# Where VectorE adds the last two output units to Y at the end of an odd step: behind both turned tiles' remainders, or each ahead of one

## The chip, the cores and the metric

One core of a Trainium2 chip runs the whole program: TensorE (PE) multiplies, VectorE (DVE), ScalarE (ACT) and GpSimd (POOL) work on its operands and results, SyncE (SP) issues the loads and stores. The metric is the device time of one execution in microseconds; three runs stand for a kernel by their median.

## The reference, cut to what matters

Attention over 4 batches of 8 heads, each 576 tokens by 64, with a second answer from a memory matrix, mixed by a gate; then two MLPs over the 2304 tokens.

```python
scores = scale * q @ k.T;  scores = where(causal, -1e9, scores)
a = exp(scores - scores.max(-1)); a /= a.sum(-1) + 1e-9
local = a @ v
q_p = where(q > 0, q, exp(q) - 1) + 1
mem_out = (q_p @ M_prev) / (q_p @ z_prev + 1e-6)
x = g * mem_out + (1 - g) * local            # g = sigmoid(beta), by head
x = (sigmoid(x @ w_gate) * (x @ w_val)) @ w_out      # 2304 x 512 -> 1536 -> 512
h = x @ w_in;  out = (h * clip(h + 3, 0, 6) / 6) @ w_out2   # 512 -> 2048 -> 512
```

## The kernel before, in words

**Numbers in two parts.** Operands of most products are cut in a part of reduced width, `hi`, and the remainder, `lo`; a product is then three matmuls (hi hi, hi lo, lo hi). ScalarE writes hi, and VectorE or GpSimd writes lo, which needs hi first.

**Pairs and steps.** The heads go in 16 pairs. A pair is two steps, p = 0 (the even step) and p = 1 (the odd one), and each step has five slots, i = 0 to 4. Pairs 0 to 4 run without MLP work (`lead`). From pair 5 on, each step carries, beside the attention of its pair, half of a quarter of the first MLP for an older batch: the function `step` on each engine. `walk` calls it: pairs 5 to 7 in a loop, pair 8 by itself with `cut` set, pairs 9 to 11 in the loop, pair 12 with `cut`, 13 and 14 in a loop, 15, and then a step pair without scores. The rest of the first MLP follows alone, and the second MLP after it.

**Turned tiles.** A head's probabilities lie by query rows. PE transposes tile i of them into PSUM (`turn_head`), ScalarE copies it to `pt_hi` (`move_hi`), and VectorE writes `pt_lo` = PSUM - `pt_hi` (`move_lo`, line 1157, counted by the semaphore `lo_done`). The table `MOVE[p][i]` says which tiles go in which slot. In the odd step's last slot, i = 4, these are tiles 2 and 3 of the even head (128x384 and 128x512); below they are m2 and m3. Tile 4 (128x320, "old") follows in slot 0 of the next step; below m4. All five must be there before PE multiplies by V (`times_v`).

**Units of the first MLP.** `FILL[p][i]` gives PE's MLP work of a slot: gate units G0 to G5, value units V0 to V5, output units O0 to O7; "T" is the turning of tile 3. A unit covers 288 tokens and accumulates in one PSUM bank. O0 to O7 take banks 6 and 7 in turn (`out_bank`), and so do the units before and after them. VectorE adds each output unit from PSUM to the running sum `Y` (line 1348, semaphore `f_y`); below s6 and s7 are those of O6 and O7. Slot (1, 4) on PE is O6, turn of tile 3, O7, scores of the next head's tile 0, turn of tile 4. The next step begins with scores of tile 1, and then G0 and G1, `times_mem`, `times_v`.

**What G0 and G1 wait for** (lines 705 to 709): G0 (t = 0) needs s6, because it takes the bank of O6, and also m2; G1 (t = 1) needs s7 and m3:

```python
if t < 2: pe.wait_ge(f_y, OU * (r + 1) - 1 + t)
if t < 2 and n is not None: pe.wait_ge(lo_done, piece_head(n - 1, 0, t + 2) + 1)
```

**Order on the engines.** It is the order of the code; each engine works its own stream in order. ScalarE in slot (1, 4): a wait for the staged weights at the end of the slot before (`high_w`, line 941), hi of tile 2, exp of tile 4 of the odd head, hi of tile 3. VectorE in slot (1, 4): mask and maximum of tile 4 of the odd head (line 1209), m2, m3, in pairs 8 and 12 also two parts of `x_lo` (`cut_x`, line 1224, each behind ScalarE's x_hi), s6, s7. The next step begins on VectorE with the mask of tile 0, the row scales (lines 1163 to 1169) and m4.

The weights arrive in a ring of three tiles: SP loads, ScalarE takes hi, GpSimd takes lo (`low_w`, line 509), which frees the tile. SP's queue in the odd step holds the loads of the next q and k, which wait for `q_s` (line 1125), ahead of the load of w_val that ScalarE waits for.

Of the kernel before, what the change touches and what calls it, by code (L numbers as in the profile page):

```python
# [31 lines left out]
def attention_and_mlps(nc, qk_t, q_n, v_n, mem, z, beta, w_gate, w_val, w_out1, w_in, w_out2, out):  # L32
# [14 lines left out]
    OU = 2 * DT  # L47
# [101 lines left out]
    with ExitStack() as ctx:  # L149
# [15 lines left out]
        def out_bank(j, alone):  # L165
            return j if alone else MLP + j % 2
# [79 lines left out]
        def softmax_tiles(p, i):  # L246
            return {2: (2, 3), 3: ()}.get(i, (i,)) if p == 0 else (i,)
# [66 lines left out]
        def tokens(c):  # L314
            return slice(c * HALF, (c + 1) * HALF)
# [804 lines left out]
        def _(dve):  # L1120
            def low_q(n, p):
                qk = qk_home(2 * n + p)
                dve.wait_ge(q_hi_done, 2 * n + p + 1)
                low = slice(D, P)
                dve.scalar_tensor_tensor(q_s[p][low, 0:S], qk[low, 0, :], SCALE, q_s[p][low, 0:S].bitcast(F32),  # L1125
                                         ALU.mult, ALU.subtract).then_inc(q_ready, 1)
# [15 lines left out]
            def move_lo(n, p, kind, i, r):  # L1142
                nn = n if p else n - 1
                if kind == "phi":
                    dve.wait_ge(hi_done, piece_phi(n, i) + 1)
                    cols = slice(0, (QT - 1) * P) if i == 0 else slice((QT - 1) * P, S)
                    src = ps[:, TURN, 0:(QT - 1) * P] if i == 0 else ps[:, turn_bank(r, 0), P:P + TAIL]
                    dst, hi = phit_lo[:, cols], phit_hi[:, cols]
                else:
                    odd = 1 - p if kind == "head" else p  # L1150
                    nn = nn if kind == "head" else n - 1
                    dve.wait_ge(hi_done, whole_bank(nn, odd, i))
                    rows = qrows[i]
                    src = ps[:, turn_bank(r, i), 0:(i + 1) * rows].rearrange("p (k c) -> p k c", c=rows)
                    cols = slice(i * P, i * P + rows)
                    hi, dst = [t[:, 0:i + 1, cols] for t in pt_main]
                dve.tensor_tensor(dst, src, hi.bitcast(F32), ALU.subtract).then_inc(lo_done, 1)  # L1157

            def row_scales(n, p):
                u, o, nn = 2 * n + p, 1 - p, (n if p else n - 1)  # L1160
                q5 = slice(0, QT)
                dve.wait_ge(exped, QT * u)
                dve.tensor_scalar(rsum_e[o][:, q5], rsum[o][:, q5], 1e-9, None, ALU.add).then_inc(sum_e, 1)
                dve.wait_ge(sum_e, u)
                dve.reciprocal(rinv[o][:, q5], rsum_e[o][:, q5]).then_inc(sum_r, 1)
                dve.wait_ge(sum_r, u)
                if known(nn, 1):
                    dve.wait_ge(normed, QT * (u - 2))
                dve.tensor_scalar(rscale[o][:, q5], rinv[o][:, q5], gate_1mg[:, bass.ds(u - 1, 1)], None, ALU.mult).then_inc(rinved, 1)  # L1169

            def phi_sum(n):
                dve.wait_ge(q_exped, n + 1)
                dve.wait_ge(relued, n + 1)
                flat = [t[:, :, :].rearrange("p t c -> p (t c)") for t in (phi, q_exp)]
                dve.scalar_tensor_tensor(flat[0], flat[1], 1.0, flat[0], ALU.min, ALU.add).then_inc(phied, 1)
# [18 lines left out]
            def low_m(n):  # L1194
                dve.wait_ge(m_hi_done, 2 * (n + 1))
                for j in two:
                    dve.tensor_tensor(m_hl[j][own(j), other(j)], m_st[own(j), :], m_hl[j][own(j), own(j)].bitcast(F32), ALU.subtract).then_inc(m_ready, 1)

            def mask_tile(n, p, j):
                u = 2 * n + p  # L1200
                if known(n, 1):
                    dve.wait_ge(turned, whole_bank(n - 1, p, j))
                dve.wait_ge(scored, QT * u + j + 1)
                settled(dve, settled_dve)
                dst = prob[p][:, p_off[j]:p_off[j] + width[j]]
                bias = mask[:, (QT - 1 - j) * P:(QT - 1 - j) * P + width[j]]
                if j == QT - 1:
                    dst, bias = [t.rearrange("p (a c) -> p a c", a=2) for t in (dst, bias)]
                dve.tensor_tensor_reduce(dst, score(p, j), bias, -1.0, MOST, ALU.add, ALU.min, nmax[p][:, j:j + 1]).then_inc(maxed, 1)  # L1209

            def x_sum(n, p, q):
                dve.wait_ge(xl_done, 2 * n + p - 1)
                dve.tensor_tensor(x_new[own(p), bass.ds(q, 1), :].rearrange("p a c -> p (a c)"), head_out(0, S)[own(p), :],
                                  x_low[own(p), :], ALU.add).then_inc(x_done, 1)
# [76 lines left out]
            def step(n, p, old, turn, scoring, r, b, q, cut):  # L1291
                alone = not (scoring or old)

                def moves(i, part=slice(None)):
                    for kind, j in MOVE[p][i][part]:
                        if (old if kind == "old" else turn):
                            move_lo(n, p, kind, j, r)

                for i in range(QT):
                    for j in softmax_tiles(p, i) if scoring else ():  # L1300
                        if j < QT - 1 or p == 1:
                            mask_tile(n, p, j)
                    if i == 0 and turn:
                        row_scales(n, p)
                    if (p, i) not in ((0, 3), (0, 4)):
                        moves(i)
                    elif i == 4:
                        moves(i, slice(0, 1))
                    if i == 1 and old:
                        x_sum(n, p, q)  # L1310
                    if p == 0 and scoring and i == 1:
                        low_q(n, 1)
                        phi_sum(n)
                    if p == 1 and turn and i == 3:
                        low_m(n)
                    if cut is not None and p == 1 and i in CUT_X:
                        cut_x(cut, CUT_X[i])
                    if p == 0 and scoring and i == QT - 2:
                        phi_scales(n)
                    for unit in FILL[p][i]:  # L1320
                        if unit[0] == "V":
                            g = int(unit[1])
                            here = slice(None), g // 2, tokens(g % 2)
                            if alone:
                                dve.wait_ge(f_gout, GV * r + g + 2)
                            else:
                                dve.wait_ge(f_sig, FQ * r + g // 2 + 1)
                            dve.wait_ge(f_val, GV * r + g + 2)
                            dve.tensor_tensor(h_val[here], h_gate[here], ps[:, unit_bank(GV + g, alone), 0:HALF], ALU.mult).then_inc(f_vout, 1)
                            if g == 0:  # L1330
                                moves(i)
                            else:
                                hidden_lo(r, g - 1)
                            if g == 2:
                                moves(i, slice(1, None))
                            if g == GV - 1:
                                if scoring:
                                    phi_scaled(n)
                                hidden_lo(r, g)
                        if unit[0] == "O":  # L1340
                            j = int(unit[1])
                            if j == 0:
                                dve.wait_ge(y_zero, B)
                            y = Y[:, j // 2, bass.ds(b * S + (j % 2) * HALF, HALF)]
                            dve.wait_ge(f_out, OU * r + j + 2)
                            if known(r, 1):
                                dve.wait_ge(f_y, OU * r + j + 1)
                            dve.tensor_tensor(y, ps[:, out_bank(j, alone), 0:HALF], y, ALU.add).then_inc(f_y, 1)  # L1348
                    if p == 0 and scoring and i == QT - 2:
                        mask_tile(n, p, QT - 1)  # L1350
                    if p == 1 and scoring and i == 1 and not is_last(n, p):
                        low_q(n + 1, 0)

            walk(dve, lead, step)


# [42 lines left out]
```

## Time and profile before

| what | value |
|---|---|
| median of 3 runs | 1146.13 us (1146.13 to 1151.61) |
| profiled execution | 1150.61 us |
| its span, first to last instruction | 1148.8 us |
| PE busy | 1099.7 us, 96% |
| VectorE busy | 580.5 us, 51% |
| ScalarE busy | 560.8 us, 49% |
| GpSimd busy | 496.9 us, 43% |
| DMA, mean | 71 GB/s |

The pairs with MLP work beside them take up the time from about 100 to 600 us of the span, some 43 us each; the second MLP starts at about 740 us. The profiled execution is 4.48 us longer than the median of the three. Busy time is that of instructions; idle time of an engine is shown with what ended it.

### The profile page before, as it was taken

To read this page: it belongs to the slowest core of one execution; us is meant where nothing else is said; L and a number is where in the kernel's file an instruction comes from. 1 tells how busy PE (TensorE), PEld (TensorE's weight loads), DVE (VectorE), ACT (ScalarE), POOL (GpSimd) and SP (SyncE) were. 2 spreads that over 40 slices of the span, in tenths; PEclk is the share of its full clock that TensorE was granted. 3 is DMA by queue.
4 is the path that set the end of the run, shared out by engine and by line. 5 is a ranking of instruction groups with operands and counts; after the bars stand their busy time and mean duration, and the time that the engine had idled before them with its cause. 6 is when DMAs were issued, how large, how long until landed. Compare 5 with 4: busy or idle time off the path is not lost.

```text
span 1148.8 us, 21924 instructions
## 1 busy us (share of the span) xinstructions
PE 1099.7 (96%) x6928; PEld 1020.3 (89%) x6928; DVE 580.5 (51%) x1313; ACT 560.8 (49%) x1259; POOL 496.9 (43%) x517
## 2 busy tenths in 40 slices
PE   4998999998999998999999999999999999999998
PEld 3677999998999998999999999899999999999996
DVE  5987656756756757756734333532323232232321
ACT  5777666675766676666753333222323232232322
POOL 5889557655756655656643444993000000000000
PEclk8999999999999999999999999899999999999999
DMA  7542432442343343343222233440000000000000
GB/s 177 138 116 51 124 99 72 115 107 61 92 114 89 99 109 87 90 117 90 57 65 74 83 82 83 125 124 28 27 0 27 0 27 0 0 27 0 27 0 27
DMA packets 100195, 81.36 MB, mean 71 GB/s; under 512 B 7729, under 2 KB 85553, under 8 KB 100145
## 3 DMA queue, kind: packets, MB, share of 16 engines
q1 hardware_dynamic: 100144, 80.77, 26.4%
q8 instruction: 22, 0.36, 0.1%
q14 instruction: 29, 0.23, 0.1%
HBM read 76.03 MB, written 4.72 MB: 70 GB/s over the span
## 4 chain that ended last, share of the span: by engine, by line
PE 81%; DVE 5%; issue 4%; DMA 3%; ACT 3%; POOL 1%; SPq 1%; DVEq 0%; ACTq 0%; POOLq 0%
PE ps L595 77%; DMA stage<-w_val 3%; PE ps L636 3%; PE ps L650 1%; DVE q_s L1125 1%; ACT pt_hi L913 1%; DVE Y L1348 1%; ACT prob L956 1%; SPq L355 1%; DVE prob L1209 1%; POOL prob L522 1%; DVE phi L1191 0%; DMA stage<-w_gate 0%; DVE znorm_e L1181 0%; DVE znorm L1179 0%
## 5 line engine op out<-in xcount | busy, mean ns | idle before, releaser
L595 PE MATMUL ps<-x_hi,WG 128*128 128x288 f32 x1536 | 326.2, 299 | 12.8 <-DVE Y L1348 11.7
L595 PEld LDWEIGHTS ps<-x_hi,WG 128*128 128x128 f32 x1536 | 252.4, 188 | 17.0 <-DVE pt_lo L1157 9.9
L595 PE MATMUL ps<-x_lo,WG 128*128 128x288 f32 x768 | 226.8, 295 | 0.0
L595 PE MATMUL ps<-c_hi,W 128*128 128x384 f32 x768 | 213.4, 340 | 2.9 <-DVE c_lo L1360 2.9
L509 POOL TENSOR_TENSOR WG<-stage,WG 128x512 fp32r<-128x512 f32 x96 | 129.1, 1363 | 125.1 <-ACT WG L941 125.1
L595 PE MATMUL ps<-W,g_hi 128*128 128x512 f32 x576 | 179.0, 391 | 0.0
L595 PE MATMUL ps<-h_hi,WO 128*128 128x288 f32 x768 | 166.2, 299 | 5.6 <-DVE Y L1348 5.6
L1365 DVE SCALAR_TENSOR_TENSOR g_raw<-g_raw,ps 128x384 f32<-128x384 f32 x96 | 53.2, 554 | 222.0 <-ACT g_raw L1101 222.0
L1101 ACT ACTIVATE g_raw<-ps 128x384 f32<-128x384 f32 x96 | 47.3, 492 | 212.3 <-PE ps L595 212.3
L595 PEld LDWEIGHTS ps<-c_hi,W 128*128 128x128 f32 x768 | 142.0, 190 | 8.0 <-DVE c_lo L1360 4.3
L522 POOL TENSOR_SCALAR prob<-prob,rscale 128x128 f32<-128x128 f32 (+4 forms) x160 | 109.1, 701 | 91.2 <-DVE rscale L1169 91.2
L595 PEld LDWEIGHTS ps<-x_lo,WG 128*128 128x128 f32 x768 | 145.0, 189 | 0.4
L595 PEld LDWEIGHTS ps<-h_hi,WO 128*128 128x128 f32 x768 | 127.4, 189 | 7.0 <-DVE Y L1348 6.6
L595 PE MATMUL ps<-c_lo,W 128*128 128x384 f32 x384 | 130.1, 339 | 0.0
L595 PEld LDWEIGHTS ps<-W,g_hi 128*128 128x128 f32 x576 | 106.9, 188 | 18.3
L956 ACT ACTIVATE prob<-prob,nmax 128x128 f32<-128x128 f32 (+4 forms) x160 | 95.9, 601 | 51.8 <-DVE nmax L1209 51.2
L595 PE MATMUL ps<-W,g_lo 128*128 128x512 f32 x288 | 113.7, 395 | 0.0
L595 PE MATMUL ps<-h_lo,WO 128*128 128x288 f32 x384 | 113.7, 296 | 0.0
L1209 DVE CUSTOM_DVE_ANT_0 prob<-ps,mask 128x128 f32<-128x128 f32 (+4 forms) x160 | 85.8, 538 | 11.3 <-PE ps L595 6.6
L1157 DVE TENSOR_TENSOR pt_lo<-ps,pt_hi 128x128 fp32r<-128x128 f32 (+4 forms) x120 | 58.6, 489 | 60.3 <-ACT pt_hi L913 60.2
L1367 DVE SCALAR_TENSOR_TENSOR g_lo<-g_raw,g_hi 128x384 fp32r<-128x384 f32 x96 | 55.9, 582 | 57.6 <-ACT g_hi L1105 57.6
L595 PE MATMUL ps<-k_hi,q_s 128*128 128x128 f32 (+2 forms) x192 | 73.7, 391 | 9.7 <-DVE k_lo L1131 8.2
(104 smaller groups left out, 1829.6 us busy)
## 6 DMA issues: line engine op xcount, KB each, us to landing
stage<-w_out SPq DMA_DIRECT2D x64, 256.0 KB, 2.8
qk_st<-qk_t SPq DMA_DIRECT2D x54, 288.0 KB, 4.3
stage<-w_gate SPq DMA_DIRECT2D x48, 256.0 KB, 3.2
stage<-w_val SPq DMA_DIRECT2D x48, 256.0 KB, 3.0
out<-y_out SPq DMA_DIRECT2D x6, 768.0 KB, 3.5
qn_st<-q_n SPq DMA_DIRECT2D x16, 256.0 KB, 3.1
stage<-w_in SPq DMA_DIRECT2D x16, 256.0 KB, 2.7
v_st<-v_n SPq DMA_DIRECT2D x12, 256.0 KB, 2.7
```

Source lines behind the costliest of these rows:

```text
L355: sp.dma_start(home[half * D:half * D + D, :, :], qk_t[bass.ds(u, 1), :, :, :].rearrange("a d c s -> (a d) c s")).then_inc(ld_qk if home i ...
L509: pool.tensor_tensor(lo, stage[k % NST][:, :], hi.bitcast(F32), ALU.subtract).then_inc(w_done, 1)
L522: pool.tensor_scalar(t, t, rscale[o][:, i:i + 1], 1.0, ALU.mult, ALU.mult).then_inc(normed, 1)
L595: return pe.matmul(o, l, r, start=start, stop=stop, skip_group_check=True)
L636: last = pe.transpose(ps[:, turn_bank(r, i), k * rows:(k + 1) * rows], prob[odd][0:rows, p_off[i] + k * P:p_off[i] + (k + 1) * P], ident[0 ...
L650: last = pe.transpose(ps[:, TURN if j == 0 else turn_bank(r, 0), o:o + rows], phi[0:rows, t, :], ident[0:rows, 0:rows])
L956: act.activation(dst, dst, ACT.Exp, scale=-1.0, bias=nmax[p][:, j:j + 1], accum_out=rsum[p][:, j:j + 1]).then_inc(exped, 1)
L1101: act.activation(g_raw[f % 2][:, :], ps[:, f % 4, 0:CH], ACT.Relu, bias=3.0).then_inc(b_relu, 1)
L1157: dve.tensor_tensor(dst, src, hi.bitcast(F32), ALU.subtract).then_inc(lo_done, 1)
L1209: dve.tensor_tensor_reduce(dst, score(p, j), bias, -1.0, MOST, ALU.add, ALU.min, nmax[p][:, j:j + 1]).then_inc(maxed, 1)
L1365: dve.scalar_tensor_tensor(raw, raw, 6.0, ps[:, f % 4, 0:CH], ALU.min, ALU.mult).then_inc(b_g, 1)
L1367: dve.scalar_tensor_tensor(g_lo[f % 4][:, :], raw, 1.0 / 6.0, g_hi[f % 4][:, :].bitcast(F32), ALU.mult, ALU.subtract).then_inc(b_lo, 1)
```

## The change

In slot i = 4 of the odd step VectorE no longer writes m2 and m3 ahead of the two sums. It adds s6, writes m2, adds s7, writes m3. The move stands behind the sum in the loop over `FILL`, and so also behind `cut_x` in pairs 8 and 12, where it stood ahead of it. Where no head is turned in that slot (the step pair behind the last pair, and the rest) nothing differs.

```diff
-                    if (p, i) not in ((0, 3), (0, 4)):
+                    if (p, i) not in ((0, 3), (0, 4), (1, 4)):
                         moves(i)
-                    elif i == 4:
+                    elif (p, i) == (0, 4):
                         moves(i, slice(0, 1))
...
                             dve.tensor_tensor(y, ps[:, out_bank(j, alone), 0:HALF], y, ALU.add).then_inc(f_y, 1)
+                            if j >= OU - 2:
+                                moves(i, slice(j - (OU - 2), j - (OU - 2) + 1))
```

VectorE, the end of an odd step in the inner loop, from the mask of tile 4 to the loop's branch, before:

```order
 L1209 ISA prob_88,nmax_93<-ps,mask 128x576
 L1209 ISA nmax_93 128x1
-L1152 REGISTER_ALU
-L1157 TENSOR_TENSOR pt_lo<-ps,pt_hi 128x3x128
-L1152 REGISTER_ALU
-L1157 TENSOR_TENSOR pt_lo<-ps,pt_hi 128x4x128
-L1345 REGISTER_ALU
-L1348 ISA
-L1348 TENSOR_TENSOR Y<-ps,Y 128x288
```

The two remainders (m2 is 128x3x128, m3 is 128x4x128) stand ahead of the first sum; the second follows it. Now:

```order
+L1345 REGISTER_ALU
+L1348 ISA
+L1348 TENSOR_TENSOR Y<-ps,Y 128x288
+L1152 REGISTER_ALU
+L1157 TENSOR_TENSOR pt_lo<-ps,pt_hi 128x3x128
+L1345 REGISTER_ALU
+L1348 ISA
+L1348 TENSOR_TENSOR Y<-ps,Y 128x288
+L1152 REGISTER_ALU
+L1157 TENSOR_TENSOR pt_lo<-ps,pt_hi 128x4x128
```

The sum of O6 has moved up past both remainders, and the sum of O7 past m3; m3 is the last instruction of the step.

VectorE, the same slot in pairs 8 and 12, where x is cut (one piece of the difference; line 1224 is the second x_lo):

```order
-L1152 REGISTER_ALU
-L1157 TENSOR_TENSOR pt_lo<-ps,pt_hi 128x3x128
-L1152 REGISTER_ALU
-L1157 TENSOR_TENSOR pt_lo<-ps,pt_hi 128x4x128
 L1223 REGISTER_ALU
 L1224 TENSOR_TENSOR x_lo<-x_new,x_hi 128x576
```

Both remainders leave their place ahead of the two x_lo and go, in turn with the sums, behind them. Nothing moves on PE, ScalarE, GpSimd or SP.

## Rows read from the trace of the kernel before

**Rows 1.** The page, costliest group: count | busy, mean ns | idle before, releaser.
```profile
L595 PE MATMUL ps<-x_hi,WG 128*128 128x288 f32 x1536 | 326.2, 299 | 12.8 <-DVE Y L1348 11.7
```

**Rows 2.** PE's timeline at the end of pair 6: start, duration, [idle before <- releaser].
```profile
185.82 0.29 PE L595 MATMUL ps<-h_hi,WO 128*128 128x288 f32 x1
...
187.46 0.30 PE L595 MATMUL ps<-h_hi,WO 128*128 128x288 f32 x1
...
188.53 0.28 PE L595 MATMUL ps<-k_lo,q_s 128*128 128x256 f32 x1
189.65 0.40 PE L595 MATMUL ps<-x_hi,WG 128*128 128x288 f32 x1 [0.84 <-DVE Y L1348]
...
192.80 0.29 PE L595 MATMUL ps<-x_hi,WG 128*128 128x288 f32 x1
```

**Rows 3.** VectorE's timeline at the same place.
```profile
185.12 0.75 DVE L1209 CUSTOM_DVE_ANT_0 prob<-ps,mask 128x576 f32<-128x576 f32 x1
...
187.21 0.56 DVE L1157 TENSOR_TENSOR pt_lo<-ps,pt_hi 128x384 fp32r<-128x384 f32 x1 [1.33 <-ACT pt_hi L913]
188.45 0.69 DVE L1157 TENSOR_TENSOR pt_lo<-ps,pt_hi 128x512 fp32r<-128x512 f32 x1 [0.68 <-ACT pt_hi L913]
189.06 0.81 DVE L1348 TENSOR_TENSOR Y<-ps,Y 128x288 f32 x2
189.97 0.29 DVE L1209 CUSTOM_DVE_ANT_0 prob<-ps,mask 128x128 f32<-128x128 f32 x1
```

**Rows 4.** ScalarE's timeline at the same place.
```profile
186.17 0.63 ACT L941 ACTIVATE WG<-stage 128x512 fp32r<-128x512 f32 x1 [2.12 <-DMA stage<-w_val]
186.70 0.47 ACT L913 ACTIVATE pt_hi<-ps 128x384 fp32r<-128x384 f32 x1
```

**Rows 5.** PE's timeline: the first product of G0 behind other pairs.
```profile
145.27 0.60 PE L595 MATMUL ps<-x_hi,WG 128*128 128x288 f32 x1 [2.39 <-DVE Y L1348]
...
279.44 0.39 PE L595 MATMUL ps<-x_hi,WG 128*128 128x288 f32 x1 [0.96 <-DVE Y L1348]
...
454.33 0.40 PE L595 MATMUL ps<-x_hi,WG 128*128 128x288 f32 x1 [1.03 <-DVE Y L1348]
...
498.24 0.39 PE L595 MATMUL ps<-x_hi,WG 128*128 128x288 f32 x1 [1.85 <-DVE Y L1348]
```

**Rows 6.** VectorE's timeline: m2 and m3 of pair 5, m2 of pair 13.
```profile
142.83 0.56 DVE L1157 TENSOR_TENSOR pt_lo<-ps,pt_hi 128x384 fp32r<-128x384 f32 x1 [2.88 <-ACT pt_hi L913]
144.07 0.69 DVE L1157 TENSOR_TENSOR pt_lo<-ps,pt_hi 128x512 fp32r<-128x512 f32 x1 [0.68 <-ACT pt_hi L913]
...
495.80 0.56 DVE L1157 TENSOR_TENSOR pt_lo<-ps,pt_hi 128x384 fp32r<-128x384 f32 x1 [2.44 <-ACT pt_hi L913]
```

**Rows 7.** VectorE's timeline, the end of pair 8 (x is cut here) and the next step's start.
```profile
278.84 0.82 DVE L1348 TENSOR_TENSOR Y<-ps,Y 128x288 f32 x2
282.26 0.29 DVE L1209 CUSTOM_DVE_ANT_0 prob<-ps,mask 128x128 f32<-128x128 f32 x1 [2.60 <-issue]
```

**Rows 8.** PE's timeline behind pair 8: products by V, and a later gate unit.
```profile
283.80 0.58 PE L595 MATMUL ps<-pt_hi,v_hl 128*128 128x128 f32 x2 [0.29 <-DVE pt_lo L1157]
...
304.12 0.40 PE L595 MATMUL ps<-x_hi,WG 128*128 128x288 f32 x1 [0.48 <-DVE h_val L1329]
```

**Rows 9.** VectorE's timeline, the end of pair 12 (x is cut here) and the next step's start.
```profile
453.74 0.81 DVE L1348 TENSOR_TENSOR Y<-ps,Y 128x288 f32 x2
454.47 0.28 DVE L1209 CUSTOM_DVE_ANT_0 prob<-ps,mask 128x128 f32<-128x128 f32 x1
```

**Rows 10.** Stretches: length, busy of PE, PEld, DVE, ACT, POOL, granted clock, DMA share.
```profile
145.00:148.00 3.00, 2.73 (x11) 2.74 (x12) 2.03 (x10) 1.75 (x4) 1.08 (x3) 0.53 0.36 100
...
499.00:503.00 4.00, 4.00 (x31) 3.93 (x30) 0.96 (x4) 3.03 (x8) 3.31 (x6) 1.00 0.05 14
```

**Rows 11.** The chain that ended last, merged: PE's first pieces behind pairs 5 and 13.
```profile
145.27 10.86 PE ps L595 x66
...
498.24 9.37 PE ps L595 x66
```

## The prediction

> **What bounds the kernel now.** I read the page first: PE is busy for 96% of the span (the table above), so only a change that removes PE's idle time or its work can shorten anything. The page's costliest group, the products of x with the gate and value weights, sat idle for 12.8 us before its instructions, and 11.7 of that was ended by a sum to Y [rows 1]. I then went through PE's timeline of the eleven pairs, 5 to 15. Each has exactly one such wait, at the first product of G0: 0.84 us behind pair 6 [rows 2], 2.39, 0.96, 1.03 and 1.85 behind pairs 5, 8, 12 and 13 [rows 5], the other six between 0.34 (pair 15) and 1.05. In a plain pair it is the only wait PE has in 43 us, so the pair is as long as PE's work and this wait.
>
> **What the wait is, in pair 6.** PE ends the scores of tile 1 at 188.81 (188.53 + 0.28) and starts G0 at 189.65 [rows 2]. VectorE is free at 185.87, when the mask of tile 4 is done (185.12 + 0.75), and then stands idle for 1.33 us until ScalarE's hi of tile 2 is there; it writes m2 from 187.21 to 187.77, waits 0.68 us for hi of tile 3, writes m3 from 188.45 to 189.14, and only then does s6 [rows 3]. ScalarE is late because it waited 2.12 us for the staged w_val; its hi of tile 2 ends at 187.17 [rows 4]. But O6 was done long before: its last matmul ends at 186.11, and that of O7 at 187.76 [rows 2]. Both sums wait in line behind remainders that wait for ScalarE. A sum takes 0.41 us from start to start (0.81 for two, 0.46 for the last), and PE starts 0.13 us after s6's end.
>
> **Part 1: s6 and m2 ahead of G0, plain pairs.** After the change s6 runs from about 186.15 to 186.6, in the idle 1.33 us, at no cost. m2 keeps its start, 187.21, since it waits for ScalarE, and ends at 187.77; with 0.13 us for the signal G0 may start at 187.90. PE comes at 188.81. The wait of 0.84 us goes whole, with 0.9 us to spare. The same holds where m2 starts about 2.4 us ahead of G0. Two pairs are different. Behind pair 5 PE comes at 142.88 (145.27 - 2.39) and m2 ends at 143.39 [rows 5, 6]: G0 at 143.52, 0.64 us of wait remain, 1.75 are gained. Behind pair 13 PE comes at 496.39 and m2 ends at 496.36: 0.10 remain, 1.75 are gained. In pair 15 the wait of 0.34 goes.
>
> Sum: 11.7 for all eleven, less 0.96 and 1.03 for pairs 8 and 12, less the 0.64 and 0.10 that remain: **9.0 us** gained in nine pairs.
>
> **Part 2: G1.** It now waits for m3. s7 can start when O7 is done, at 187.80, and ends by 188.26; m3 starts as before at 188.45, with ScalarE's hi, and ends at 189.14. G1 starts when G0's work is done: the two units fill 189.65 to 193.09, less a little at the end [rows 2], so a unit is 1.6 us, and G1 starts at 188.81 + 1.6 = 190.4. That is 1.3 us after m3. In pair 5 m3 ends at 144.76 and G1 comes at 143.52 + 1.6 = 145.1: closer, still nothing. Cost zero; the cover is G0's own work.
>
> **Part 3: what stands behind m3.** The mask of tile 0 started at 189.97, behind s7; now it follows m3, at about 189.2, 0.77 us sooner [rows 3]. PE is 0.84 us sooner. So VectorE, and ScalarE's exp and GpSimd's scaling that hang on it, keep step with PE to within 0.1 us. Only behind pairs 5 and 13 does PE run ahead of them by a further 1.0 us. What such a lag costs can be read behind pair 8, where the mask comes 2.8 us after G0's start (282.26 against 279.44), not 0.3 as in pair 6: PE loses 0.29 and 0.48 us there [rows 7, 8]. A lag of 1.0 against one of 2.5 that costs 0.77: between 0 and 0.3 us each. I take 0: pair 6, with the mask 0.3 us behind G0, loses nothing, and the lag here is nearer to it than to pair 8's.
>
> **Part 4: pairs 8 and 12, a loss.** Here m2 and m3 were written while ScalarE made x_hi, in time that VectorE otherwise waits. They now come behind both x_lo. In pair 8, s6 still starts at 278.84 [rows 7]. m2 is queued between it and s7 (0.48 us from start to start) and m3 behind s7 (0.61): VectorE ends the step 1.1 us later. Behind that the next mask comes 1.1 us later, and m4 too, so the products by V start at 284.9 in place of 283.80 [rows 8]. They waited already, so PE loses the full **1.1 us**; G0's own 0.5 us is inside that. The work through GpSimd and the staging that ends in the wait at 304.12 is later by the same 1.1 and adds nothing. In pair 12 the mask starts 0.14 us behind G0 and not 2.8 (454.47 against 454.33) [rows 5, 9], so 1.1 us more leaves it well short of pair 8's lag, and only G0's part counts: s6 starts at 453.74, m2 ends 0.94 us later at 454.68, G0 at 454.81 in place of 454.33: **0.5 us**. Ends of this term: 0.5 each (1.0) to 1.1 each (2.2); I take 1.6.
>
> **Part 5: TensorE's clock.** Behind the longest wait, 2.39 us at pair 5, the granted clock is 0.53 from 145 to 148, that is near the lower level of 1.2 GHz; behind 1.85 us at pair 13 it stays at 1.00, 2.4 GHz [rows 10]. The same 66 matmuls take 10.86 us behind pair 5 and 9.37 behind pair 13 [rows 11]. So a wait cut to 0.64 us may also give back 1.5 us. I leave it out of the forecast: the profiled execution is 4.5 us longer than the median, and such a slow stretch is one of the few things in it that could be absent from the two equal runs at 1146.13.
> The Trainium skill, page "TensorE: Matmul & The Clock Gate", Part 1: The HAM clock gate, says that the default state is throttled and that activity releases it. The trace agrees here (0.53, then 0.92 and 1.00), and by that rule the 1.5 us would be gained.
>
> **Sum.** 9.0 - 1.6 = **7.4 us**. Against the profiled execution that is 1150.6 - 7.4 = 1143.2 (1141.7 with the clock). Against the median, 1146.13 - 7.4 = **1138.7 us**, 0.65% less.
>
> **Rivals.**
> *The long waits are not in the median run.* The waits behind pairs 5 and 13 exceed the usual 0.85 us by 1.5 and 1.0. In the shorter runs ScalarE's weights may come on time there. Then these two give 0.85 each and not 1.75: 7.4 - 1.8 = 5.6, **1140.5 us**. For it: the 4.5 us between the executions. Against it: pair 5 is the first with MLP work, so its wait may be in every run.
> *The clock as well*: 8.9, **1137.2 us**.
> *The wait moves on.* PE runs ahead and meets ScalarE or GpSimd one unit later, at the copy of G0 or the products by V. If half of every wait came back, 4.5 - 1.6 = 2.9: **1143.2 us**. Against it: 1.3 us of slack at G1.
> *Slower: m3 is held by O7.* VectorE now stands at s7 until O7 is done, with m3, the next mask, the row scales and all of GpSimd's scaling in line. The Trainium skill, same page, Architectural detail, says that VectorE's queue is strict FIFO; the rows below agree in that no sum overtook a remainder. It decides where O7 ends more than about 0.3 us after ScalarE's hi of tile 3: then m3 ends later than s7 did. If that held in all eleven pairs with pair 8's price of 1.1 us, 12 us would be lost: **1158 us**. Against it: O7 ends at 187.76 and m3's operand is there at 188.4; only in pair 15 are the two about even.
> *No effect*: G0 is in truth held by something that s6 only happens to end with. 1146.1. Against it: PE follows s6 by 0.13 us.
>
> **How the numbers follow.** Forecast 0.56; without the long waits 0.17; with the clock 0.10; the wait moves on 0.10; slower 0.04; no effect 0.03. A measurement of this kernel tells some 0.5% (5.7 us, 1140.4) from no change. The forecast, the clock and about a third of the rival at 1140.5 lie below that: faster 0.72; same 0.24; slower 0.04. The range: down to the clock's case with the loss of Part 4 at its low end and a little over (1137.2 - 0.6, and 1 us for the spread of runs), 1135.6; up to the wait that moves on, 1143.2, so 1143.6.
>
> **What the profile after would show.** On PE's timeline G0 follows the scores without a wait behind nine pairs (0.6 behind pair 5 at most), and pairs are 0.8 us shorter. On VectorE one sum stands in the former idle time ahead of m2, and m3 keeps its distance to ScalarE's hi. Behind pair 8 the wait before the products by V is about 0.9 us, and behind pair 12 G0 waits 1.5. I am wrong if a new wait shows at G1, at `times_v` in plain pairs, or if the sum of O6 ends behind hi of tile 2.

## The result, and the profile after

The changed kernel takes 1140.53 us (median of 10 runs, 1137.47 to 1143.73), the kernel before, beside it, 1147.58 us (median of 10, 1145.89 to 1151.61). The ratio is 0.9931, 95% interval 0.9917 to 0.9944. By the medians that is 7.05 us less, by the ratio 7.9, where 7.4 was forecast; the time itself is 1.8 us above the forecast 1138.7, mostly because the kernel before is now 1.45 us above the 1146.13 that the forecast started from. In two later comparisons the kernel before took 1146.83 and 1147.75 us.

The page after, the busy time of the engines and PE's costliest group, to be read against [rows 1]:

```profile
span 1139.1 us, 21924 instructions
...
PE 1099.2 (96%) x6928; PEld 1020.8 (90%) x6928; DVE 587.2 (52%) x1313; ACT 560.2 (49%) x1259; POOL 498.6 (44%) x517
...
L595 PE MATMUL ps<-x_hi,WG 128*128 128x288 f32 x1536 | 325.5, 298 | 3.9 <-DVE pt_lo L1157 2.7
```

Of 12.8 us of idle time before these products 3.9 are left, and what ends them is no longer a sum to Y but a remainder: 2.7 us, which are two waits, 1.28 and 1.39 us, behind pairs 8 and 12.

At the end of pair 6, VectorE after (start, duration, idle before), to be read against [rows 3]:

```profile
182.87 0.46 DVE L1348 TENSOR_TENSOR Y<-ps,Y 128x288 f32 x1 [0.39 <-PE ps L595]
183.70 0.56 DVE L1157 TENSOR_TENSOR pt_lo<-ps,pt_hi 128x384 fp32r<-128x384 f32 x1 [0.37 <-ACT pt_hi L913]
184.50 0.46 DVE L1348 TENSOR_TENSOR Y<-ps,Y 128x288 f32 x1 [0.25 <-PE ps L595]
184.94 0.69 DVE L1157 TENSOR_TENSOR pt_lo<-ps,pt_hi 128x512 fp32r<-128x512 f32 x1
185.88 0.29 DVE L1209 CUSTOM_DVE_ANT_0 prob<-ps,mask 128x128 f32<-128x128 f32 x1 [0.25 <-issue]
```

s6 stands alone in the former idle time, m2 waits for ScalarE as before, s7 waits 0.25 us for O7, and m3 follows it. m3 starts 1.24 us behind m2, as before (188.45 against 187.21 [rows 3]), so s7 does not delay it. PE at the same place, and then at V4, the first unit of the odd step, and at the G0 behind pair 7:

```profile
185.14 0.27 PE L595 MATMUL ps<-k_lo,q_s 128*128 128x256 f32 x1
185.25 0.30 PE L595 MATMUL ps<-x_hi,WG 128*128 128x288 f32 x1
...
207.05 0.30 PE L595 MATMUL ps<-x_hi,WG 128*128 128x288 f32 x1
...
227.01 0.30 PE L595 MATMUL ps<-x_hi,WG 128*128 128x288 f32 x1
```

G0 starts 0.11 us after the start of the last score matmul; it had been 1.12 us, 188.53 to 189.65 [rows 2]. The same two units, V4 and the G0 behind pair 7, before:

```profile
211.55 0.30 PE L595 MATMUL ps<-x_hi,WG 128*128 128x288 f32 x1
...
232.74 0.39 PE L595 MATMUL ps<-x_hi,WG 128*128 128x288 f32 x1 [1.05 <-DVE Y L1348]
```

From the G0 behind pair 6 to the one behind pair 7 it was 232.74 - 189.65 = 43.09 us and is now 227.01 - 185.25 = 41.76.

Where the time went, from the start of V4 in the odd step of one pair to the start of V4 in the next pair (each row holds the odd step, the wait at the G0 behind it, and the next even step):

| behind pair | before, us | after, us | difference | wait in the row before |
|---|---|---|---|---|
| 5 | 46.62 | 42.76 | -3.86 | 2.39, and a slower clock behind it |
| 6 | 42.89 | 41.77 | -1.12 | 0.84 |
| 7 | 43.09 | 41.76 | -1.33 | 1.05 |
| 8 (x cut) | 47.25 | 47.96 | +0.71 | 0.96 |
| 9 | 43.42 | 42.48 | -0.94 | 0.74 |
| 10 | 42.79 | 41.76 | -1.03 | 0.74 |
| 11 | 42.92 | 41.78 | -1.14 | 0.89 |
| 12 (x cut) | 45.22 | 47.08 | +1.86 | 1.03 |
| 13 | 43.90 | 41.78 | -2.12 | 1.85 |
| 14 | 42.87 | 41.77 | -1.10 | 0.86 |
| 15 | 39.65 | 39.27 | -0.38 | 0.34 |

The sum is -10.45. The stretch ahead of it was 0.48 us longer in this execution and the one behind it 0.3, which leaves the 9.7 us between the spans of 1148.8 and 1139.1.

Of the wait of 2.39 us behind pair 5, 0.10 is left in this execution (the last score matmul ends at 143.28, G0 starts at 143.38), too short for a bracket. Both columns hold slow stretches of TensorE's clock, 1.5 us each: before in rows 5 and 8, after in rows 8 and 12. That of row 8 stands behind another wait, at O4 in slot 2, which the change doesn't touch; more on it below.

The pairs where x is cut lost. VectorE behind pair 8 before, m3 and the two x_lo that follow it at once:

```profile
276.90 0.69 DVE L1157 TENSOR_TENSOR pt_lo<-ps,pt_hi 128x512 fp32r<-128x512 f32 x1 [1.53 <-ACT pt_hi L913]
277.51 1.42 DVE L1224 TENSOR_TENSOR x_lo<-x_new,x_hi 128x576 fp32r<-128x576 f32 x2
```

And after, to be read against [rows 7] as well:

```profile
271.63 1.43 DVE L1224 TENSOR_TENSOR x_lo<-x_new,x_hi 128x576 fp32r<-128x576 f32 x2 [2.66 <-ACT x_hi L948]
272.97 0.45 DVE L1348 TENSOR_TENSOR Y<-ps,Y 128x288 f32 x1
273.34 0.55 DVE L1157 TENSOR_TENSOR pt_lo<-ps,pt_hi 128x384 fp32r<-128x384 f32 x1
273.80 0.45 DVE L1348 TENSOR_TENSOR Y<-ps,Y 128x288 f32 x1
274.17 0.68 DVE L1157 TENSOR_TENSOR pt_lo<-ps,pt_hi 128x512 fp32r<-128x512 f32 x1
277.12 0.29 DVE L1209 CUSTOM_DVE_ANT_0 prob<-ps,mask 128x128 f32<-128x128 f32 x1 [2.27 <-issue]
```

VectorE idles for 2.66 us until x_hi is there, time in which both remainders used to be written, and writes them behind it. PE, after, behind pairs 8 and 12 (G0, the products by V, G0), with [rows 5, 8]:

```profile
273.94 0.40 PE L595 MATMUL ps<-x_hi,WG 128*128 128x288 f32 x1 [1.28 <-DVE pt_lo L1157]
...
278.66 0.58 PE L595 MATMUL ps<-pt_hi,v_hl 128*128 128x128 f32 x2 [0.64 <-DVE pt_lo L1157]
...
446.43 0.45 PE L595 MATMUL ps<-x_hi,WG 128*128 128x288 f32 x1 [1.39 <-DVE pt_lo L1157]
```

The waits grew from 0.96, 0.29 and 1.03 us. Behind pair 12 the clock fell as well in this execution. The stretches after (length, busy of PE, PEld, DVE, ACT, POOL, granted clock, DMA share, GB/s):

```profile
446.00:450.00 4.00, 3.57 (x15) 3.58 (x16) 2.77 (x11) 2.12 (x5) 1.46 (x4) 0.58 0.00 0
450.00:454.00 4.00, 4.00 (x28) 3.91 (x28) 0.00 (x0) 2.27 (x7) 3.83 (x6) 0.99 0.00 0
```

0.58 is near 0.5, the lower level of 1.2 GHz. The step behind that G0 takes 23.44 us, and 21.91 before: 1.53 of the 1.86.

### The profile page after: what moved, and what is told of

Read it like the earlier page. It is cut to its first block, busy times and chain, and to the rows that moved or that the text cites. A ratio compares the mean times of both kernels' runs of the same rounds, so it can differ in the third digit from the quotient of the medians.

```text
span 1139.1 us, 21924 instructions
## 1 busy us (share of the span) xinstructions
PE 1099.2 (96%) x6928; PEld 1020.8 (90%) x6928; DVE 587.2 (52%) x1313; ACT 560.2 (49%) x1259; POOL 498.6 (44%) x517
## 4 chain that ended last, share of the span: by engine, by line
PE 85%; DVE 4%; issue 3%; ACT 2%; POOL 2%; DMA 1%; DVEq 0%; SPq 0%; ACTq 0%; POOLq 0%
PE ps L595 81%; PE ps L636 3%; PE ps L650 1%; POOL prob L522 1%; DMA stage<-w_gate 1%; DVE prob L1209 1%; DVE phi L1191 0%; DMA stage<-w_val 0%; POOL WO L509 0%; ACT pt_hi L913 0%; DVE znorm_e L1181 0%; DVE Y L1348 0%; DVE znorm L1179 0%; ACT prob L956 0%; DVE q_s L1125 0%
## 5 line engine op out<-in xcount | busy, mean ns | idle before, releaser
L1369 DVE SCALAR_TENSOR_TENSOR g_lo<-g_raw,g_hi 128x384 fp32r<-128x384 f32 x96 | 60.4, 630 | 57.5 <-ACT g_hi L1105 57.5
L1329 DVE TENSOR_TENSOR h_val<-h_gate,ps 128x288 f32<-128x288 f32 x96 | 42.9, 447 | 74.7 <-PE ps L595 53.9
```

Of the source, the lines that this page charges most:

```text
L1369: dve.scalar_tensor_tensor(g_lo[f % 4][:, :], raw, 1.0 / 6.0, g_hi[f % 4][:, :].bitcast(F32), ALU.mult, ALU.subtract).then_inc(b_lo, 1)
```

## The experiments

**Theory A**: the gain is PE's wait at G0 in nine plain pairs, each worth its idle time plus a fixed part; the change loses in pairs 8 and 12. **Rivals**: the cut pairs cost nothing (B); the gain is steadier loads and a steadier clock in one execution or the other, not the order (C).

### Only the plain pairs, only the cut pairs

```diff
-                    if (p, i) not in ((0, 3), (0, 4), (1, 4)):
+                    if (p, i) not in ((0, 3), (0, 4), (1, 4)) or ((p, i) == (1, 4) and cut is not None):
...
-                            if j >= OU - 2:
+                            if j >= OU - 2 and cut is None:
```

> The order of the change in the plain pairs only; pairs 8 and 12, where x is cut, keep the order of before (m2, m3, x_lo, x_lo, s6, s7). Theory A: the gain is PE's wait at G0 in nine plain pairs, each the idle time of its row plus some 0.26 us (a stream of matmuls overlaps by 0.16 us and starts again 0.10 us late), and the two cut pairs lose 0.7 and 0.3 us, and 1.5 more where the clock falls. Then this kernel is 1 to 2.5 us shorter than the change and 8 to 9.5 us shorter than before, and behind pairs 8 and 12 G0 waits 0.96 and 1.03 us again as before. Rival B: the cut pairs cost nothing and the change's gain is all in place already: same as the change within 0.3 us.

Measured: 1137.32 us (4 runs) beside 1146.83 before (19 runs), ratio 0.9917 (0.9889 to 0.9946): 9.5 us less, at the upper end of the 8 to 9.5 expected. Its interval overlaps that of the change, so by itself it doesn't show that the cut pairs cost anything. The second kernel has `cut is None` and `cut is not None` exchanged:

> The complement: the order of the change only in pairs 8 and 12, the plain pairs as before. Theory A: 1.0 us longer than before, up to 2.5 where the clock falls behind one of them; every plain pair keeps its wait (0.74 to 1.05 us) and its odd half of 21.0 us. Rival C (the gain comes from steadier loads or a steadier clock over the whole stretch and not from the order in each pair): shorter than before by some us, with plain pairs changed too.

Measured: 1150.23 us (10 runs), ratio 1.0030 (1.0014 to 1.0047): 3.4 us more, clear of no change, and more than the 1.0 to 2.5 expected. The two add to -6.1, the whole change is -7.05. The rows of pairs 6 and 7 (V4 to V4) are 41.78 us each in the first kernel and 42.87 and 43.07 in the second, as after and before. So B and C both fall: the order in the plain pairs is the gain, and the cut pairs cost, which the second kernel shows. G0 behind pairs 8 and 12 in the first, and behind pair 12 in the second with the clock of the stretch behind it:

```profile
272.79 0.39 PE L595 MATMUL ps<-x_hi,WG 128*128 128x288 f32 x1 [1.03 <-DVE Y L1348]
...
445.84 0.39 PE L595 MATMUL ps<-x_hi,WG 128*128 128x288 f32 x1 [0.94 <-DVE Y L1348]
```

```profile
453.70 0.40 PE L595 MATMUL ps<-x_hi,WG 128*128 128x288 f32 x1 [1.39 <-DVE pt_lo L1157]
```

```profile
455.00:460.00 5.00, 5.00 (x29) 4.93 (x29) 1.08 (x5) 3.29 (x8) 4.09 (x7) 0.74 0.00 0
```

In the second kernel's trace the cut pairs are 0.68 us (pair 8) and 1.84 us (pair 12, 1.52 of it clock) longer than before, 2.5 in all; the other 0.9 us of its median isn't placed. A lower clock over the runs may be part of it: the mean granted clock of its ten runs is 0.9920, that of the nineteen before 0.9939, an estimated 2.2 us of the span where the cut pairs of the trace have 1.52, but single runs scatter from 0.987 to 0.997.

### Both sums first

```diff
-                            if j >= OU - 2:
-                                moves(i, slice(j - (OU - 2), j - (OU - 2) + 1))
+                            if j == OU - 1:
+                                moves(i)
```

> Both sums first and then both remainders (s6, s7, m2, m3), in all eleven pairs. m2 now waits behind s7, which waits for O7. In pair 6 by the rows of before: s7 187.80 to 188.26, m2 to 188.75, G0 at 188.88 where PE comes at 188.65 to 188.81. Theory A with its fixed part: a wait of only 0.1 to 0.25 us still costs the fixed 0.26 us, so each plain pair is 0.35 to 0.5 us longer than with the change: 3 to 4.5 us longer than the change, 2.5 to 4 shorter than before. If a wait costs only the idle time in its row: 1 to 2 us longer than the change.

Measured: 1144.06 us (10 runs), ratio 0.9973 (0.9961 to 0.9985): 2.8 us less than before, 3.5 more than the change by the medians, both as theory A had it. VectorE and PE behind pair 6, and PE at the next V4 and the next G0:

```profile
185.38 0.46 DVE L1348 TENSOR_TENSOR Y<-ps,Y 128x288 f32 x1 [0.38 <-PE ps L595]
187.01 0.46 DVE L1348 TENSOR_TENSOR Y<-ps,Y 128x288 f32 x1 [1.18 <-PE ps L595]
187.38 1.15 DVE L1157 TENSOR_TENSOR pt_lo<-ps,pt_hi 128x384 fp32r<-128x384 f32 x2
```

```profile
187.65 0.27 PE L595 MATMUL ps<-k_lo,q_s 128*128 128x256 f32 x1
187.99 0.40 PE L595 MATMUL ps<-x_hi,WG 128*128 128x288 f32 x1
...
209.88 0.30 PE L595 MATMUL ps<-x_hi,WG 128*128 128x288 f32 x1
...
230.09 0.40 PE L595 MATMUL ps<-x_hi,WG 128*128 128x288 f32 x1
```

This is the fixed part seen alone. The row of 187.99 counts only 0.07 us of idle time (187.65 + 0.27 to 187.99), yet G0 starts 0.34 us after the last score matmul's start, not 0.11, and its first matmul takes 0.40 us, not 0.30. From this G0 to the next it is 230.09 - 187.99 = 42.10 us against 41.76: 0.34 us lost for 0.07 counted. m2 now hangs on O7, by way of s7, and that is what taking sums and remainders in turn avoids.

### m2 first, and m3 ahead of x_lo

```diff
-                    elif (p, i) == (0, 4):
+                    elif i == 4:
                         moves(i, slice(0, 1))
+                        if p == 1:
+                            out_sum(OU - 2)
+                            moves(i, slice(1, 2))
```

The diff is against the changed kernel and cut to what matters: `out_sum(j)` is the sum of line 1348 with its waits (line 1306 in the rows below); the loop over `FILL` leaves j = 6 out and no longer holds the moves.

> m2, s6, m3, s7 in all pairs, with m3 ahead of both x_lo in pairs 8 and 12 and s7 behind them. s6 fills the 0.68 us between m2 and m3, m3 starts as before. Theory A: plain pairs as with the change (s6 ends by 188.2 in the times of pair 6, PE comes at 188.7), except behind pair 5, where G0 may wait some 0.4 us more; in pairs 8 and 12 m2 and m3 are back in the time in which VectorE waits for x_hi, s6 too, so G0 starts 0.4 us sooner than before instead of 0.33 later. 1.4 to 2.5 us shorter than the change, 8.5 to 10 shorter than before. Rival (the whole loss of the cut pairs was the clock, or none): same as the change.

Measured: 1138.07 us (4 runs), ratio 0.9919 (0.9890 to 0.9947): 8.8 us less than before, as expected. VectorE and PE behind pair 8:

```profile
270.46 0.55 DVE L1157 TENSOR_TENSOR pt_lo<-ps,pt_hi 128x384 fp32r<-128x384 f32 x1
271.30 0.46 DVE L1306 TENSOR_TENSOR Y<-ps,Y 128x288 f32 x1 [0.29 <-issue]
271.96 0.69 DVE L1157 TENSOR_TENSOR pt_lo<-ps,pt_hi 128x512 fp32r<-128x512 f32 x1 [0.20 <-ACT pt_hi L913]
272.57 1.42 DVE L1224 TENSOR_TENSOR x_lo<-x_new,x_hi 128x576 fp32r<-128x576 f32 x2
```

```profile
274.24 0.40 PE L595 MATMUL ps<-x_hi,WG 128*128 128x288 f32 x1 [0.77 <-DVE x_lo L1224]
```

G0 there waits for x_lo now, 0.77 us and not 1.28. Behind pair 12 it is 0.91 and not 1.39, and behind pair 5 0.95 where e8_change_again has 0.49, as expected. Against the kernel before G0 gains only 0.19 and 0.12 us of wait in the cut pairs, where 0.4 was expected. Between this kernel, the change and e1_plain_only the intervals decide nothing. There is also a new wait, 0.89 us for x_lo, at the first unit behind the last step pair; it is read below, at e6_m2_first_x_lo_late.

### ScalarE's hi of tile 2 behind the exp

```diff
-                    early = MOVE[p][i] if i < QT - 1 else MOVE[p][i][:1]
+                    early = MOVE[p][i] if i < QT - 1 else MOVE[p][i][:1 - p]
```

> The changed kernel, but ScalarE takes the exp of the odd head's tile 4 ahead of the hi of tile 2 and not behind it. hi of tile 2, and with it m2, comes 0.86 us later; hi of tile 3 stays. The prediction gave m2 0.9 us to spare ahead of G0, and m3 1.3 us ahead of G1. If so, plain pairs stay within 0.3 us of the change each (G0 at the edge, with the fixed 0.26 us in some): 0 to 3 us longer than the change. If PE was in fact held by m2 already, each pair is 0.9 us longer, 8 to 10 us in all.

Measured: 1141.81 us (7 runs) beside 1147.75 before (15 runs), ratio 0.9954 (0.9939 to 0.9969). VectorE's m2 and PE's G0 behind pair 6:

```profile
186.00 0.56 DVE L1157 TENSOR_TENSOR pt_lo<-ps,pt_hi 128x384 fp32r<-128x384 f32 x1 [1.11 <-ACT pt_hi L913]
```

```profile
186.70 0.27 PE L595 MATMUL ps<-k_lo,q_s 128*128 128x256 f32 x1
186.81 0.30 PE L595 MATMUL ps<-x_hi,WG 128*128 128x288 f32 x1
```

m2 ends at 186.56, 0.25 us ahead of G0, and PE goes on without a gap. The odd step of the plain pairs is as long as with the change (19.98 us), but for pair 13 (20.38) and pair 5. So the 0.9 us to spare were there, and m2 did not hold PE. In the cut pairs G0 waits 1.76 us, where it is 1.31 and 1.30 with the change. The median is 2.8 us above that of the change beside it (e8_change_again), but the intervals overlap, and the pairs in the two traces differ by 0.4 us only; what the rest is stays open.

### The change again

> The changed kernel once more, beside the others on the same chip: 6 to 8 us shorter than before; the odd half of a plain pair 19.97 us. If the clock falls behind pair 12 in this execution too, the even half of pair 13 is 23.4 us and not 21.9.

Measured: 1139.03 us (5 runs), ratio 0.9937 (0.9917 to 0.9957): 8.7 us less by the medians, 7.2 by the ratio, where 6 to 8 was expected. G0 behind pair 5:

```profile
143.18 0.40 PE L595 MATMUL ps<-x_hi,WG 128*128 128x288 f32 x1 [0.49 <-DVE pt_lo L1157]
```

The forecast had 0.64 us left of the wait there; here it is 0.49. In the first profile after it was 0.10, since PE came 0.4 us later relative to m2. The even step of pair 13 takes 21.89 us this time: in pair 12 the clock fell ahead of G0, behind the wait at O4, and not behind G0.

### A version that takes the same mechanism further

With the plain-pairs order, the two x_lo of slot 2 also go behind the sums of their slot (the second piece of the diff stands behind the loop over `FILL`). PE waits 1.98 us there in each cut pair, at O4, for the sum of O2, which stands behind x_lo; after the change, in pair 8:

```profile
264.22 0.40 PE L595 MATMUL ps<-h_hi,WO 128*128 128x288 f32 x1 [1.98 <-DVE Y L1348]
```

```diff
-                    if cut is not None and p == 1 and i in CUT_X:
+                    if cut is not None and p == 1 and i == 4:
                         cut_x(cut, CUT_X[i])
...
+                    if cut is not None and p == 1 and i == 2:
+                        cut_x(cut, CUT_X[i])
```

> The kernel with the plain pairs' new order only (e1_plain_only), and in slot 2 of the odd step, where x is cut as well, both x_lo behind the sums of O2 and O3 instead of ahead. In the rows after the change PE waits 1.98 us there for O2's sum behind pairs 8 and 12, 0.21 and 1.42 in the last step pair. The same mechanism as in the change: a sum stands in line behind work that waits for ScalarE. Theory A, with 0.26 us of fixed cost for each wait: 2.2 us for each of pairs 8 and 12, 1.5 to 1.9 in the last, and up to 1.5 where the clock fell behind the wait: 5.5 to 8 us shorter than e1_plain_only, 15 to 17 shorter than before. Rival: the wait moves to the gate units of the next step, since x_lo comes some 1 us later in part; then 2 to 4 us.

Measured: **1131.89 us** (5 runs), ratio 0.9863 (0.9843 to 0.9883): 15.9 us less than before and 7.1 less than the change run beside it, the fastest of all these kernels; 15 to 17 less than before was expected. VectorE in slot 2 of pair 8, and PE's waits at O4 and at G0:

```profile
262.33 0.45 DVE L1348 TENSOR_TENSOR Y<-ps,Y 128x288 f32 x1
263.00 0.46 DVE L1348 TENSOR_TENSOR Y<-ps,Y 128x288 f32 x1 [0.22 <-PE ps L595]
263.44 1.74 DVE L1224 TENSOR_TENSOR x_lo<-x_new,x_hi 128x576 fp32r<-128x576 f32 x2
```

```profile
267.04 0.40 PE L595 MATMUL ps<-h_hi,WO 128*128 128x288 f32 x1 [0.72 <-DVE Y L1348]
272.54 0.39 PE L595 MATMUL ps<-x_hi,WG 128*128 128x288 f32 x1 [1.34 <-DVE Y L1348]
```

The wait of 1.98 us is gone. 0.72 of it comes back later in the pair, at O6, and G0 waits 0.3 us longer than in e1_plain_only, 0.4 behind pair 12; probably since x_lo and the mask of tile 3 still have to be done. In this execution the clock doesn't fall at all between 100 and 600 us.

The time is as expected, the way there is not. Expected was 2.2 us for each cut pair. The rows (V4 to V4) of pairs 8 and 12 are 45.08 and 44.28 us, against 45.85 and 46.66 in e1_plain_only, and 1.45 of the latter is a fall of the clock. So the order gives 0.8 and 0.9 us a pair, of which 0.2 and 0.3 are lost again in the next pair's row, and some 0.5 in the last step pair. Against e8_change_again the pairs are 5.0 us shorter, and two falls of the clock that are not there make some 3.0 of it. The mean granted clock of the runs points the same way: 0.997 here (5 runs), 0.995 in e1_plain_only (4), 0.993 in e8_change_again (5). How much of the 15.9 us every run would owe to fewer falls isn't shown.

> The same move of both x_lo in slot 2, on e4_m2_s6_m3_s7. Theory A: as much as in e5_x_lo_late, so within 1 us of it; G0 behind pairs 8 and 12 waits 0.2 us less than there.

Measured: 1134.26 us (6 runs), ratio 0.9888 (0.9870 to 0.9906). It was expected within 1 us of the last one and is 2.4 above. G0 behind pairs 8 and 12 waits 1.03 and 1.17 us and not 1.34, as expected. In the profiled executions the pairs themselves are 1.0 us shorter (464.5 against 465.4 us from V4 in pair 5 to V4 in the last step pair) and the stretch behind is 2.3 us longer (546.4 against 544.1). In that stretch the two differ in the place of one sum, s6, ahead of or behind the last two x_lo. VectorE and PE there, in this kernel:

```profile
602.85 0.46 DVE L1306 TENSOR_TENSOR Y<-ps,Y 128x288 f32<-128x288 f32 x1 [1.18 <-PE ps L595]
603.23 1.42 DVE L1224 TENSOR_TENSOR x_lo<-x_new,x_hi 128x576 fp32r<-128x576 f32 x2
```

```profile
604.89 0.39 PE L595 MATMUL ps<-x_hi,WG 128*128 128x288 f32 x1 [0.88 <-DVE x_lo L1224]
```

Here s6 waits 1.18 us for O6 with x_lo, which could have been written, in line behind it, and PE then waits 0.88 us for x_lo. In e5_x_lo_late the x_lo stand ahead of s6 and PE has no such wait; V4 to the next unit G0 takes 17.23 us there and 18.29 here. It is the mechanism of this document turned round, and 1.06 of the 2.3 us. The rest isn't placed; how much the stretch varies without any difference is told below. In the cut pairs themselves m2 first is 0.2 to 0.3 us a pair better by these two traces; it costs where no tile is turned.

## Why the prediction was right

**Where G0's wait comes from, and that it goes**: right. s6 stands in the idle time, m2 and not s6 frees G0, and PE goes on without a wait behind the plain pairs. The distance of m2 from G0, 0.9 us, was confirmed by e7_hi_late, and that G1 has cover by the absence of any wait at G1.

**The size of a wait**: too small, and this is the first term that was off. The forecast took a wait at its idle time, 0.84 for pair 6. The table has 1.12. Pairs 6, 7, 10, 11, 13 and 14 exceed their idle time by 0.24 to 0.29, pair 9 by 0.20; only pair 15 by no more than 0.04. So some 0.27 us is a fixed part: a matmul that follows without a gap starts 0.11 us after the one before it though that one lasts 0.27, and the first matmul behind a gap takes 0.10 longer. e3_both_sums_first shows it alone. The nine plain pairs gave 13.0 us in the two traces, 11.5 without the slow clock behind pair 5, against a forecast of 9.0; 0.6 of the 2.5 is pair 5, where 0.10 us of the wait was left in this execution and not 0.64.

**Part 3, that nothing behind m3 is late**: right. The mask of tile 0 comes 0.63 us after G0's start in pair 6, 0.3 us later than before and not the 0.1 of the forecast, and no new wait shows: the even steps behind the plain pairs 6 to 14 take 21.80 us each, and 21.87 to 21.90 before.

**The loss in pairs 8 and 12**: the mechanism was right, the sizes were not, and a part was missing. G0 is 0.32 and 0.36 us later, not 0.5, since m2 starts 0.37 us behind s6 and not 0.48. The mask behind pair 8 is 0.74 us later relative to x_lo (277.12 - 271.63 = 5.49 against 282.26 - 277.51 = 4.75), not 1.1: the pause marked "issue" shrank from 2.60 to 2.27. So the term without the clock is 1.04 and not 1.6. With the clock it is 2.57 in the trace, and the kernel with the cut pairs alone measures 3.4.

**The clock**: the forecast considered only that the slow stretch behind pair 5 might go, and left it out. It did go, but another came behind pair 12, so each trace holds two between 100 and 600 us and the clock gave nothing between them. Not to ask what the clock does behind the waits that grow was the omission. That the longer wait brought the fall behind pair 12 isn't shown, only likely. Where G0 waits 1.3 us or more there, the clock fell behind it in four of six profiles (after, e2, e3, e7); in e8_change_again, the same kernel, it fell already behind the wait at O4, and in e5_x_lo_late not at all. Where G0 waits 1.17 us or less (before, e1, e4, e6) it never fell there, though in e1_plain_only it fell at O4. And a slow stretch isn't decided by the wait ahead of it. Behind pair 5 the cut-only kernel waits 2.42 us, as long as before, and the clock stays at 1.00:

```profile
145.39 0.39 PE L595 MATMUL ps<-x_hi,WG 128*128 128x288 f32 x1 [2.42 <-DVE Y L1348]
```

```profile
145.00:148.00 3.00, 2.61 (x19) 2.62 (x20) 2.15 (x10) 1.94 (x5) 0.96 (x3) 1.00 0.37 101
```

**The sum**: 7.05 for 7.4. That it came so near is luck: a gain that was 2.5 us too small and a loss that was up to 1.8 us too small err in opposite ways. 11.5 - 3.4 is 8.1; the last 1.0 us isn't placed. The 9.7 us between the two profiled spans is no measure of the change either, since the profiled execution before was 3.0 us above its median and the one after 0.4. The rival without the long waits at 1140.5 has the measured time, but not by its mechanism: pair 5's wait of 2.4 us came again in the cut-only kernel, while pair 13's was 1.14 there and not 1.85. With the fixed part and the clock taken into account, e1_plain_only was expected at 8 to 9.5 less and measured 9.5.

**The slower rival**, m3 held by O7, didn't occur: s7 waits 0.25 us for O7 behind pair 6, and m3 keeps its 1.24 us from m2. e3_both_sums_first shows what such a hold costs when it is m2 that is held: 0.34 us a pair.

Dropping G0's wait for m2 wasn't tried: by the code it also keeps what PE writes behind G0 and G1 from the turned tiles' banks until they have been read.

## What to carry to other kernels

An engine that works in order should do first what is ready and waited for; here a sum stood in line behind remainders that waited for a third engine. The order that is right in the common case was wrong in the two pairs where that engine's idle time had held the work that moved: look for the variants of a step in which the cover is used, and leave them out. The same goes for the last step pair of e6_m2_first_x_lo_late, where a sum moved ahead of x_lo had itself to wait. And in a stream of matmuls like this one, count an idle gap of TensorE at some 0.27 us more than its row says.

## What the runs showed of the hardware

**A short wait costs more than its row.** 0.07 us of counted idle time cost 0.34 us a pair; 0.84 cost 1.12. A row counts idle time from the end of the matmul before, and in a stream the next one starts 0.16 us ahead of that end.

**The clock's falls are not bound to a wait.** Between 100 and 600 us, where each fall costs some 1.5 us, the ten profiles hold 2 (before), 2 (after), 1, 2, 2, 1 (e1 to e4), 0, 0 (e5, e6), 2 (e7) and 2 (e8). Each came during a wait of 1.39 us or more or within 2 us of its end, but waits of 2.42, 1.99 and 1.85 us passed without one, and the two kernels whose longest waits there are 1.34 and 1.17 us have none. At the start of the second MLP PE waits 1.87 us in both of these traces; the clock holds in the first, e1_plain_only (726 to 731), and falls in the second, after (728 to 733):

```profile
726.00:731.00 5.00, 3.61 (x18) 2.97 (x19) 3.48 (x4) 0.57 (x2) 4.83 (x6) 1.00 0.37 116
```

```profile
728.00:733.00 5.00, 3.71 (x12) 2.88 (x13) 3.06 (x4) 0.49 (x1) 4.83 (x6) 0.69 0.43 109
```

The stretch from V4 in the last step pair to the end is 543.8 us in e1_plain_only and 546.4 after, with the same order of instructions. The Trainium skill, page "TensorE: Matmul & The Clock Gate", Part 1: The HAM clock gate, says of the start of a kernel that the number of matmuls at the lower rate varies from run to run. These traces show it in the middle of the program too: in two executions of one kernel the clock fell behind G0 of pair 12 (after) or behind O4 of pair 12 (e8_change_again). So 1.5 us steps in one trace are no evidence for or against an order of instructions, and a difference of 2 us between two kernels needs their runs.
